# A fused fp32 attention and two-layer MLP kernel: GpSimd takes four weight sums, the inverse row sums are stored and loaded in another order, and the units of the first MLP layer overlap

## The reference

```python
scores = scale * np.matmul(q, k.transpose(0, 1, 3, 2))
scores = cap * np.tanh(scores / cap)
scores = scores - np.max(scores, axis=-1, keepdims=True)
attn = np.exp(scores)
attn = attn / (np.sum(attn, axis=-1, keepdims=True) + 1e-09)
x = np.matmul(attn, v)            # then (B, S, H*D)
...
h = x @ w_in
g = np.where(h > 0.0, h, np.exp(np.minimum(h, 0.0)) - 1.0)
x = g @ w_out                     # moe
...
h = x @ w_in
g = np.maximum(0.01 * h, h)
return g @ w_out                  # moe2
```

## Time and profile before

| | us |
|---|---|
| median of three runs | 575.67 |
| the profiled execution, whole | 574.71 |
| its span, first to last instruction | 572.9 |
| TensorE busy | 556.7 (97% of the span, 2908 matmuls) |
| VectorE busy | 469.4 (82%) |
| ScalarE busy | 352.8 (62%) |
| GpSimd busy | 275.2 (48%) |

### The profile page before, as it was taken

One profiled execution on the slowest core, in us unless ns is written; L12 is line 12 of the kernel. 1 busy time (PEld: TensorE's weight loads), 2 busy tenths in 40 slices (PEclk: granted clock), 3 DMA queues, 4 the chain that ended last, 5 costly groups with the idle time before them and its releaser, 6 DMA issues.

```text
span 572.9 us, 8610 instructions
## 1 busy us (share of the span) xinstructions
PE 556.7 (97%) x2908; PEld 499.4 (87%) x2908; DVE 469.4 (82%) x758; ACT 352.8 (62%) x606; POOL 275.2 (48%) x273
## 2 busy tenths in 40 slices
PE   6999989999999999999999999989999999999997
PEld 5777779889998999999999999879999998999997
DVE  5899998878875133898988999889999779999881
ACT  6999988999995455654644454536454445544440
POOL 6779998799965655552000003856666530000000
DMA  6455564455423333335644332031113225536251
GB/s 174 106 143 128 150 174 125 123 130 146 98 65 89 98 112 110 111 108 165 213 135 158 131 99 67 1 110 56 57 55 90 77 84 192 159 119 220 84 170 51
DMA packets 34172, 67.07 MB, mean 117 GB/s; under 512 B 6864, under 2 KB 18768, under 8 KB 34128
## 3 DMA queue, kind: packets, MB, share of 16 engines
q1 hardware_dynamic: 33984, 66.28, 39.4%
q10 hardware_dynamic: 144, 0.23, 0.1%
HBM read 63.70 MB, written 2.80 MB: 116 GB/s over the span
## 4 chain that ended last, share of the span: by engine, by line
PE 77%; DVE 10%; ACT 4%; issue 3%; POOL 3%; DMA 2%; ACTq 0%; SPq 0%; DVEq 0%; POOLq 0%
PE mlp_ps L1129 8%; PE mlp_ps L1131 8%; PE mlp_ps L1130 8%; PE o_ps L1129 6%; PE o_ps L1131 6%; PE o_ps L1130 6%; PE scores L1129 4%; PE scores L1130 4%; PE scores L1131 4%; PE probs_t L1103 4%; PE probs_t L1131 4%; PE probs_t L1130 4%; PE probs_t L1129 4%; PE scores L1088 2%; PE o_ps L1122 2%
## 5 line engine op out<-in xcount | busy, mean ns | idle before, releaser
L559 POOL TENSOR_TENSOR w_lo<-w_raw,w_hi 128x768 fp32r<-128x768 f32 (+1 forms) x62 | 104.2, 1681 | 62.3 <-ACT w_hi L621 61.9
L559 POOL TENSOR_TENSOR w_lo<-s_sum,w_hi 128x384 fp32r<-128x384 f32 x32 | 38.8, 1228 | 114.5 <-ACT w_hi L621 114.5
L621 ACT ACTIVATE w_hi<-s_sum 128x768 fp32r<-128x768 f32 (+1 forms) x64 | 43.4, 684 | 76.6 <-DVE s_sum L880 51.9
L621 ACT ACTIVATE w_hi<-w_raw 128x768 fp32r<-128x768 f32 (+1 forms) x77 | 56.5, 737 | 31.1 <-PE o_ps L1131 15.7
L601 ACT ACTIVATE soft<-soft,neg_max 112x448 f32<-112x448 f32 x96 | 63.6, 673 | 1.8 <-DVE soft L758 1.7
L758 DVE TENSOR_SCALAR_CACHE_REDUCE soft<-soft,neg_abs 112x448 f32<-112x448 f32 x96 | 60.9, 671 | 2.2 <-ACT soft L591 1.9
L1129 PE MATMUL mlp_ps<-x_hi,w_hi 128*128 128x448 f32 x132 | 49.2, 373 | 0.4 <-issue 0.4
L765 DVE TENSOR_TENSOR p_lo<-probs_t,p_hi 112x896 fp32r<-112x896 f32 x37 | 40.3, 1089 | 10.0 <-ACT p_hi L610 9.9
L1130 PE MATMUL mlp_ps<-x_lo,w_hi 128*128 128x448 f32 x132 | 48.2, 365 | 0.0
L1131 PE MATMUL mlp_ps<-x_hi,w_lo 128*128 128x448 f32 x132 | 48.2, 365 | 0.0
L591 ACT ACTIVATE soft<-scores 112x896 f32<-112x896 f32 x47 | 43.4, 924 | 6.0 <-PE scores L1089 5.9
(11 more groups left out here) (238 smaller groups left out, 1747.7 us busy)
## 6 DMA issues: line engine op xcount, KB each, us to landing
w_raw<-w_units SPq DMA_DIRECT2D x120, 384.0 KB, 3.2
q_raw<-qT SPq DMA_DIRECT2D x24, 224.0 KB, 3.1
k_raw<-kT SPq DMA_DIRECT2D x23, 224.0 KB, 3.0
v_raw<-v_rows SPq DMA_DIRECT2D x24, 112.0 KB, 3.2
inv_all<-inv_rows SPq DMA_DIRECT2D x24, 112.0 KB, 3.4
y_t<-y_out SPq DMA_DIRECT2D x12, 224.0 KB, 2.8
inv_rows<-row_inv SPq DMA_DIRECT2D x24, 1.8 KB, 3.1
k_raw<-kT ACTq DMA_DIRECT2D x1, 224.0 KB, 3.1
```

The source lines that it names most:

```text
L559: pool.tensor_tensor(w_part(w_lo, n), w_source(n), f32(w_part(w_hi, n)), ALU.subtract).then_inc(w_lo_pool, 1)
L621: nc.scalar.activation(w_part(w_hi, n), w_source(n), ACT.Copy).then_inc(w_hi_done, 1)
```

## The change

Six edits, all in the order of work; the arithmetic is the same, and every matmul is kept.

1. SyncE: in step 2h+3 it now issues the store of head h's inverse, then a first-layer weight load if there is one, then v, then the load of that inverse, and in the next step k and q. Before, the store came in step 2h+4 behind k and q, and the load in step 2h+5.
2. VectorE scales O of head h (h below 8) in step 2h+6, before 2h+7.
3. The first three high weights on VectorE move from steps 12, 16, 20 to 11, 15, 19, and their low parts on GpSimd from the end of steps 13, 17, 21 to the end of steps 12, 16, 20.
4. Chunks: step 30 has one chunk in place of three, step 54 has ten of the last place in place of eight, and the list `LATER` makes unit u start before unit u-1 has its last chunk, up to unit 11; units 12 to 15 are in a row.
5. The four weight sums of block 0 go from VectorE to GpSimd (`first_block_sum`), ahead of GpSimd's first low weights of the blocks.
6. At the border VectorE's list is reordered: both x sums first, and `x_low("p2")` with the x sum for p4 stand ahead of the block adds. ScalarE's `x_high("p2")` comes before the loop over the blocks.

```diff
-         29: ((2, (3,)),), 30: ((0, (4,)), (1, (4,)), (2, (4,)))}
+         29: ((2, (3,)),), 30: ((0, (4,)),)}
-         52: (0, 0, 6), 53: (0, 0, 6), 54: (0, 0, 8)}
+         52: (0, 0, 6), 53: (0, 0, 6), 54: (0, 0, 10)}
-LATER = [(0, 5), (1, 5), (3, 0), (3, 1), (2, 5)] + [(u, c) for u in range(3, MAT_UNITS) for c in range(KC) if u > 3 or c > 1]
+LATER = [(0, 5), (1, 4), (1, 5), (3, 0), (2, 4), (3, 1), (3, 2), (3, 3), (2, 5), (3, 4)] + [
+    chunk for u in range(4, 12) for chunk in [(u, c) for c in range(4)] + [(u - 1, 5), (u, 4)]] + [(11, 5)] + [
+    (u, c) for u in range(12, MAT_UNITS) for c in range(KC)]
...
             for s in range(STEPS):
                 for u in units_ending_at(s - 1):
                     load_w(u + AHEAD + RAW)
+                if s % 2 == 1 and 0 <= (s - 3) // 2 < NHEAD:
+                    store_inv((s - 3) // 2)
+                if s in FIRST_LOADS:
+                    load_w(FIRST_LOADS.index(s))
+                if s % 2 == 1 and 2 <= s // 2 + 1 < NHEAD:
+                    load_v(s // 2 + 1)
+                if s % 2 == 1 and 0 <= (s - 3) // 2 < NHEAD:
+                    load_inv((s - 3) // 2)
                 if s % 2 == 0 and s // 2 + 4 < NHEAD:
                     load_k(s // 2 + 4)
                     load_q(s // 2 + 4)
-                if s % 2 == 1 and 0 <= (s - 5) // 2 < NHEAD:
-                    load_inv((s - 5) // 2)
-                if s % 2 == 1 and 2 <= s // 2 + 1 < NHEAD:
-                    load_v(s // 2 + 1)
-                if s % 2 == 0 and 0 <= (s - 4) // 2 < NHEAD:
-                    store_inv((s - 4) // 2)
-                if s in FIRST_LOADS:
-                    load_w(FIRST_LOADS.index(s))
...
+            def first_block_sum(p):
+                n = GEMM1 + BLOCK_AT[0, p]
+                raws = ITEM_RAWS[n]
+                for r in raws:
+                    pool.wait_ge(*loaded(r))
+                pool.wait_ge(*split_done(GEMM1 - 9))
...
+                pool.tensor_tensor(dst, *args).then_inc(s_pool_done, 1)
...
-                if s in (13, 17, 21):
-                    split_w((s - 13) // 4)
+                if s in (12, 16, 20):
+                    split_w((s - 12) // 4)
             for n in LO_ON_POOL[units_ending_at(STEPS - 1)[0] + AHEAD:]:
+                if n == GEMM1:
+                    for p in SUMS:
+                        first_block_sum(p)
                 split_w(n)
...
             w_high(GEMM1 + 7)
+            x_high("p2")
...
-                if i == 0 and p == "p1":
-                    x_high("p2")
...
-                if s in (12, 16, 20):
-                    w_high((s - 12) // 4)
-                if s % 2 == 1 and 0 <= (s - 7) // 2 < DIRECT:
-                    scale_o((s - 7) // 2)
+                if s in (11, 15, 19):
+                    w_high((s - 11) // 4)
+                if s % 2 == 0 and 0 <= (s - 6) // 2 < DIRECT:
+                    scale_o((s - 6) // 2)
...
             second(0)
-            for p in SUMS:
-                weight_sum(GEMM1 + BLOCK_AT[0, p])
-
-            weight_sum(GEMM1 + BLOCK_AT[1, "p5"])
-            weight_sum(GEMM1 + BLOCK_AT[1, "p6"])
             x_low("p1")
             dve.wait_ge(xc_split, X_GROUPS.index("p1") + 1)
             x_sum(y12, y12, y11, ALU.subtract)
+            x_sum(y11, y22, y11, ALU.add)
+
+            weight_sum(GEMM1 + BLOCK_AT[1, "p5"])
+            x_low("p5")
+            weight_sum(GEMM1 + BLOCK_AT[1, "p6"])
+            x_low("p6")
             weight_sum(GEMM1 + BLOCK_AT[1, "p3"])
-            x_low("p5")
-            x_sum(y11, y22, y11, ALU.add)
             weight_sum(GEMM1 + BLOCK_AT[1, "p7"])
-            x_low("p6")
             dve.wait_ge(u3_done, HC)
             add_to(0, "p4", y21, kept_u2[0], y21_done)
+            x_low("p2")
+            dve.wait_ge(xc_split, X_GROUPS.index("p2") + 1)
+            x_sum(y21, y21, y11, ALU.subtract)
             for q in range(GEMM1 + 1, GEMM2[1] + 1):
...
-                if i == 0 and p == "p6":
-                    x_low("p2")
                 if p == "p6":
                     block_add(i, "p6")
...
-                    dve.wait_ge(xc_split, X_GROUPS.index("p2") + 1)
-                    x_sum(y21, y21, y11, ALU.subtract)
```

More of the change, by code:

```diff
@@ L1 @@
 from contextlib import ExitStack
+import itertools
 import numpy as np
@@ L74, in chunks_at @@
     for n in MIXED.get(s, (0, 0, 0)):
[L75 to L78, removed]
+        runs = itertools.groupby(LATER[done:done + n], lambda chunk: chunk[0])
+        places.append([(u, [c for _, c in run]) for u, run in runs])
         done += n
@@ L156 @@
 SUM_ITEMS = ([n for n in range(GEMM1) if item_name(n)[1] in SUMS]
-             + [GEMM1 + BLOCK_AT[i, p] for i in range(HF) for p in SUMS]
+             + [GEMM1 + BLOCK_AT[i, p] for i in range(1, HF) for p in SUMS]
              + [n for n in range(GEMM2[1], ITEMS) if item_name(n)[1] in SUMS])
@@ L316, in build @@
         relu_done, act_done, g_done = sem("relu_done"), sem("act_done"), sem("g_done")
-        s_done = sem("s_done")
+        s_done, s_pool_done = sem("s_done"), sem("s_pool_done")
         t1_done, t2_done, t3_done, t4_done = (sem(f"t{i}_done") for i in range(1, 5))
@@ L372, in sum_done @@
         def sum_done(n):
+            if item_name(n)[0] == "blocks" and item_name(n)[2] == 0:
+                return s_pool_done, SUMS.index(item_name(n)[1]) + 1
             return s_done, SUM_ITEMS.index(n) + 1
@@ L559, in split_w @@
                 pool.tensor_tensor(w_part(w_lo, n), w_source(n), f32(w_part(w_hi, n)), ALU.subtract).then_inc(w_lo_pool, 1)
+            def first_block_sum(p):
[4 more added lines that the diff above has]
+                pool.wait_ge(*split_done(GEMM1 - 9))
+                dst, (lo, hi) = w_source(n), (slice(0, HALF), slice(HALF, UNIT))
+                if p == "p6" or p == "p3":
+                    ahead = GEMM1 + BLOCK_AT[0, SUMS[SUMS.index(p) - 1]]
+                    pool.wait_ge(*sum_done(ahead))
+                    before = w_source(ahead)
+                a11, a12 = w_raw[:, raws[0] % RAW, lo], w_raw[:, raws[0] % RAW, hi]
+                if p == "p5":
+                    args = a11, a12, ALU.add
+                elif p == "p7":
+                    args = a11, w_raw[:, raws[1] % RAW, lo], ALU.subtract
+                elif p == "p6":
+                    args = before, a11, ALU.subtract
+                else:
+                    args = a12, before, ALU.subtract
+                pool.tensor_tensor(dst, *args).then_inc(s_pool_done, 1)
             pool.memset(zero[:, :], 0.0).then_inc(zero_set, 1)
```

## The result

Twenty runs of the changed kernel took 576.09 to 581.83 us, median 577.49; twenty of the kernel before, median 574.69. The ratio is 1.0062, 95% interval 1.0049 to 1.0074: 3.6 us slower (2.8 to 4.3). This ratio is the estimate of the timed runs; the two medians lie 2.8 us apart and the two means 3.3. The forecast was +3.5 us, or 579.2 us on the older median of 575.67. The profiled execution is one of the slower ones: 580.33 us, span 578.5, against 574.71 and 572.9. The two traces must therefore account for 5.6 us.

A forecast was written before the change was run, and what follows sets the result against it. TensorE, busy 97% of the span, was taken as the bound, with a different engine binding each part. -0.9 + 0.1 + 0.45 + 3.9 = +3.5 us on 575.67 gave 579.2 us, range 573.2 to 581.8.

The forecast's parts named there:

- the clock, which the prediction had as a rival: TensorE's clock falls to 1.2 of 2.4 GHz in the border's new stop: +2.5 us, 581.7 us, chance 0.10.
- the sign it named itself: If the slices behind the border's new stop show a lower clock, the rival of a falling TensorE clock holds.
- A: Inverse, scale_o and moved low weights (edits 1 to 3): waits for x_raw go, v comes later; -0.9 us, bounds -2.0 to +0.7.
- the values start 0.3 to 0.7 us later: Head 5's values start that much later than 47.89, waiting for v in place of x_raw; 0.4 us charged.
- B: Chunk tables (edit 4): 1.13 us gained, 1.22 given back in step 54; +0.1 us, bounds -1.2 to +1.2.
- C: Units 10 and 11 end in step 51, so unit 13's low weights arrive late: +0.45 us, bounds 0 to +1.0.
- D: Border (edits 5 and 6): VectorE's chain lengthens and (1,p3) starts later; +3.9 us, bounds -2.2 to +5.5.
- the wait of 1.39 stays: On VectorE's border chain, x_low("p2") still waits 1.39 us for ScalarE's high part.
- 4.8 - 2.33 + 1.47: Delay of the first block add: net meetings, less four sums off VectorE, plus the y21 sum; given as +3.9 to +4.3.
- 11 meetings: At the border, VectorE instructions colliding with GpSimd's w_lo, 0.98 us each: 10.5 us with the four sums, against 5.7 before.
- (0,p6) was not later: At the border, the forecast had (0,p6), at 368.28 before, wait about 0.5 us more.
- TensorE now stands about 5: At (1,p3), TensorE's stop was to grow from 1.38 us to about 5 us, with its clock at 1.00.

The follow-up runs named there:

- the product computed twice: The changed kernel with TensorE computing product (1,p6), ahead of the stop at (1,p3), twice into the same bank, nine matmuls more: 1.0020 against the kernel before.
- The sums back on VectorE: The changed kernel with edit 5 undone, VectorE forming the four weight sums right behind second(0): 1.0059 against the kernel before, +3.4 us.
- ScalarE's high part first: The changed kernel with ScalarE making x_high("p1") before the first two high weights of the blocks: 1.0045 against the kernel before, +2.6 us.
- the longer stop: The kernel before with VectorE making x_low("p2") twice ahead of the block adds: 1.0051, +2.9 us.
- the y21 sum late: The changed kernel with the sum of y21 again behind the first block adds: 0.9997 against the kernel before, -0.2 us.
- edits 1 and 2 alone: The kernel before with only SyncE's order for the inverse and O scaled one step sooner: 0.9993, -0.4 us.
- the adds first: The kernel before with VectorE's first block adds and block_hidden of (0,p3) and (0,p7) moved ahead of x_low("p2"): 0.9965, -2.0 us.

## Why the prediction was right, and where not

**The time** was right: +3.5 forecast, +3.6 (2.8 to 4.3) measured. That it fits so closely is luck. The forecast held that the clock stays at 1.00, and with the clock up the whole kernel is +1.2 us (the product computed twice, 1.0020, 1.0000 to 1.0039) to +1.8 us (the executions of the changed kernel without a fall, see below), a third to a half of the forecast; the rest came from the clock, which the prediction had as a rival. By the sign it named itself, a lower clock behind the stop, that rival holds. What carried the direction was right: the y21 sum delays the bank of (0,p3).

**A** was right in sign and place: no wait for `x_raw`, v in its stead. The size was -0.6 for -0.9. That "the values start 0.3 to 0.7 us later" was right at its upper end (49.06 for 47.89, less 0.5 of a later start). Two sizes in it were off and partly cancel: the gain on VectorE was 0.7 us (65.2 to 64.5 without the moved low weights) where I had 1.30, and the delay of v cost 0.2 where I had 0.4.

**B and C** were right, in each wait named: +0.2 for +0.1, +0.5 for +0.45.

**D.** Right: the bank of (0,p3) decides, freed by a chain on VectorE; the y21 sum ahead of the adds is on it (2.2 us with its meeting, predicted 1.47 and a meeting); the wait of 1.39 stays (1.40). The first block add came at 376.78, 3.5 us later than before; 0.6 of that lies ahead of the border, so it is 2.9 where 4.3 was predicted. Wrong in it:
- The sum itself. 4.8 - 2.33 + 1.47 is 3.9 and not 4.33; and 11 meetings at 0.98 are 10.8 us and not 10.5. With 10.8 the sum gives 4.2.
- "I count 11 meetings to 377 ... against 5.7 before". Of VectorE's instructions up to the adds seven met a `w_lo`, as many as before. Beside the sums only two did (1.36 for 0.95 and 1.90 for 1.08, so +1.2 where I had 3.3). GpSimd was the one that waited: its first sum took 3.65 us.

```profile
345.62 3.65 POOL L587 TENSOR_TENSOR s_sum<-w_raw 128x384 f32<-128x384 f32 x1 [82.11 <-DMA w_raw<-w_units]
349.44 1.01 POOL L587 TENSOR_TENSOR s_sum<-s_sum,w_raw 128x384 f32<-128x384 f32 x1 [0.17 <-POOL s_sum L587]
```

- In the place of the missing meetings came a wait that I had not seen, 2.68 us for `x_high("p1")`. The order showed it: `w_high` of the sums stands ahead of it on ScalarE. With it the chain is 0.6 (shift) + 1.2 + 2.7 - 2.3 + 2.2 - 0.9 (one meeting fewer, and less) = 3.5.
- (0,p6) was not later, and the stop at (1,p1) was not foreseen: it takes the bank that the adds of y21 free, and those ended 1.9 us later than before (371.6).
- "TensorE now stands about 5": it stood 3.1 us and 1.2 us, the second ahead of the first.

**The clock** was priced as a rival, 0.10, with +2.5 us; in the trace TensorE ran at half for 5.8 us and it cost 2.66. It did not take the place of the forecast but came on top of a border 1.5 us cheaper than forecast. That "no run here shows such a fall" was true, and the chance was too low: what speaks for it is that the new stop was to be more than three times the longest in this stretch.

**What stays open.** The clock did not fall in every execution of the changed kernel. The profiled one has a mean granted clock of 0.993; of the twenty, eleven have 0.997 or less (median 578.95 us) and nine 0.999 or 1.000 (median 576.53 us, 1.8 above the kernel before). The sums back on VectorE show it in 7 of 11, ScalarE's high part first in 9 of 12, the longer stop in all ten, the y21 sum late in 3 of 12, the product computed twice in none of 12. In the kernel before it is 3 in 29, 3 in 35 and 3 in 22 on three chips, so some falls come without a long stop. Why a stop of 3.1 us is followed by a fall in one execution and not in the next is open; the mean does not say where in an execution the clock fell. One of the slowest (581.43) has 1.000, so the clock does not explain all of the spread.

## What to carry to other kernels

Price a stop of TensorE twice: its length, and what the clock loses behind it; here an instruction of 2.25 us cost 3.7. The second part is a risk and not a fixed price: in the changed kernel about half of the executions paid it. Of an instruction moved ahead on an engine, ask what it now stands in front of, not only what it waits for: the same engine gained 2.0 us from the opposite move. And when a wait on a chain is taken away while its instructions and another engine's hold each other up, look whether more such meetings fill the gap (2.7 us less wait, 0.25 us gained).

## What the runs showed of the hardware

**Slow stretches at a granted clock of 1.00.** Sixty-three matmuls of 448 columns took 13.02 us here in the kernel before, 12.77 in the changed one: 0.2067 against 0.2027 us each.

```profile
396.56 0.37 PE L1131 MATMUL mlp_ps<-p_hi,w_lo 128*128 128x448 f32 x1
...
409.58 0.37 PE L1131 MATMUL o_ps<-p_hi,w_lo 128*128 128x448 f32 x1
```

```profile
401.95 0.36 PE L1159 MATMUL mlp_ps<-p_hi,w_lo 128*128 128x448 f32 x1
...
414.72 0.36 PE L1159 MATMUL o_ps<-p_hi,w_lo 128*128 128x448 f32 x1
```

Where such a stretch lies differs from profile to profile: some 90 us from 383 on in the kernel before, from 475 to the end in the changed one, both together with edits 1 and 2 alone, and none from 180 us on with the adds first. Each 90 us are worth 1.7 us. They cancel in the account above, and must not be read as an effect of an edit. Their cause is open.

**VectorE and GpSimd do not always take turns.** GpSimd's first sum, from 345.62 to 349.27 where such a sum takes 1.01 alone, overlaps three of VectorE's instructions that follow each other without a gap, and ended 1 us after VectorE turned to adds with an input in PSUM.

```profile
344.97 0.95 DVE L915 TENSOR_TENSOR w_lo<-w_raw,w_hi 128x768 fp32r<-128x768 f32 x1
345.84 1.08 DVE L869 TENSOR_TENSOR g_first<-b,g_first 128x896 fp32r<-128x896 f32 x1
346.84 1.55 DVE L926 TENSOR_TENSOR p_lo<-y,p_hi 128x1344 fp32r<-128x1344 f32 x1
348.31 0.61 DVE L922 TENSOR_TENSOR y<-p_first,mlp_ps 128x448 f32<-128x448 f32 x1
```

From 349.9 on instructions of both are longer than alone (VectorE's 1.36 and 1.90 above, GpSimd's 1.52 and 1.85). So what a meeting costs, and whom, differs; that it depends on whether the other engine leaves a gap is my reading of these rows, and no run tests it.
